# Attention mask built from rows for each bit on GpSimd, without the two bucket products

## What is computed

```
q_bits = (einsum('bhsd,dk->bhsk', q, proj) > 0)        # k_bits likewise
mask   = q_bucket[:, :, :, None] == k_bucket[:, :, None, :]
scores = scale * matmul(q, k.T)
scores = where(mask, scores, -1e9);  scores -= max(scores)
attn   = exp(scores);  attn /= attn.sum() + 1e-9
out    = matmul(attn, v)
```

## Time and profile before

| | |
|---|---|
| runs of the kernel | median 616.67 us (616.35 to 617.31), 3 runs |
| the profiled execution | 616.41 us, span of its instructions 614.7 us |
| granted TensorE clock | 1.000 of full speed |
| busy share of the span | TensorE 98%, its weight loads 82%, VectorE 70%, ScalarE 57%, GpSimd 57% |
| attention stage | from the start to about 240 us |

### The profile page before, as it was taken

The page is one execution under the profiler, slowest core; times in us unless marked ns, Lnnn a source line. Parts: engine busy times, 40 slices in busy tenths (PEclk is TensorE's granted clock), DMA queues, the critical chain, the costliest instruction groups (busy, mean ns, idle before and its releaser), DMA issues.

```text
span 614.7 us, 10917 instructions
## 1 busy us (share of the span) xinstructions
PE 605.4 (98%) x3676; PEld 503.5 (82%) x3676; DVE 431.1 (70%) x689; ACT 347.6 (57%) x700; POOL 349.3 (57%) x337
## 2 busy tenths in 40 slices
PE   7899999999999999999999999999999999999998
PEld 3667777776776776999888999999999999988887
DVE  3988888888888885788676666545677666579920
ACT  3877777777777785354444444335444444264232
POOL 4533434333337756146458988873999999234140
PEclk9999999999999999999999999999999999999999
DMA  6842323233232210001212122113222221100202
GB/s 137 244 118 64 91 66 91 64 90 90 64 90 79 62 46 3 1 2 53 69 51 69 56 64 61 60 57 99 69 85 85 86 86 51 35 1 0 86 19 102
DMA packets 27650, 42.20 MB, mean 69 GB/s; under 512 B 3425, under 2 KB 15713, under 8 KB 27617
## 3 DMA queue, kind: packets, MB, share of 16 engines
q1 hardware_dynamic: 25648, 37.38, 20.9%
q0 software_dynamic: 1728, 4.02, 2.6%
q10 hardware_dynamic: 240, 0.39, 0.3%
HBM read 38.63 MB, written 3.15 MB: 68 GB/s over the span
## 4 chain that ended last, share of the span: by engine, by line
PE 95%; DVE 2%; DMA 1%; ACT 1%; POOL 1%; issue 0%; ACTq 0%; POOLq 0%
PE banks L1882 22%; PE banks L1914 16%; PE banks L1667 12%; PE banks L1684 11%; PE banks L1734 10%; PE banks L1996 5%; PE banks L2012 5%; PE banks L1873 4%; PE banks L1707 2%; PE banks L1818 2%; PE banks L1620 2%; DMA k_raw<-in_k 1%; PE banks L1742 1%; PE banks L1858 1%; PE banks L1626 1%; PE banks L1792 1%
## 5 line engine op out<-in xcount | busy, mean ns | idle before, releaser
L1246 DVE TENSOR_REDUCE row_min<-banks 128x1 f32<-128x768 f32 x96 | 91.8, 956 | 31.8 <-PE banks L1667 31.1
L873 ACT ACTIVATE prob<-banks,row_min 128x768 f32<-128x768 f32 x96 | 87.1, 907 | 29.0 <-DVE row_min L1246 28.9
L1506 DVE TENSOR_TENSOR partial_sums<-banks,partial_sums 128x384 f32<-128x384 f32 x78 | 43.4, 557 | 54.9 <-PE banks L1914 54.7
L1734 PE MATMUL banks<-ident,prob 128*128 128x128 f32 x576 | 79.2, 273 | 1.4 <-ACT probT L374 1.4
L1734 PEld LDWEIGHTS banks<-ident,prob 128*128 128x128 f32 x576 | 68.1, 140 | 6.7 <-issue 1.9
L606 POOL TENSOR_TENSOR k_b<-k_raw,k_a 64x768 fp32r<-64x768 f32 x16 | 29.3, 1829 | 70.7 <-ACT k_a L856 70.7
L1684 PE MATMUL banks<-probT,v_in 128*64 128x384 f32 x384 | 69.0, 494 | 0.0
L1882 PE MATMUL banks<-h_hi,w_hi 128*128 128x512 f32 (+1 forms) x256 | 66.1, 339 | 0.0
L1882 PE MATMUL banks<-h_hi,w_lo 128*128 128x512 f32 (+1 forms) x256 | 65.6, 337 | 0.0
L1882 PE MATMUL banks<-h_lo,w_hi 128*128 128x512 f32 (+1 forms) x256 | 65.3, 336 | 0.0
L374 ACT COPY probT<-banks 128x384 f32<-128x384 f32 x104 | 49.1, 480 | 22.4 <-PE banks L1734 22.1
(11 more groups left out here) (216 smaller groups left out, 1515.0 us busy)
## 6 DMA issues: line engine op xcount, KB each, us to landing
w_stage<-in_moe_w_ch SPq DMA_DIRECT2D x38, 256.0 KB, 2.6
q_raw<-in_q SPq DMA_DIRECT2D x32, 192.0 KB, 3.3
k_raw<-in_k SPq DMA_DIRECT2D x30, 192.0 KB, 3.6
w_pair<-in_moe_w_ch SPq DMA_DIRECT2D x7, 512.0 KB, 3.7
v_in<-in_v SPq DMA_DIRECT2D x16, 192.0 KB, 2.8
w_stage<-in_moe_w_ch SPq DMA_DIRECT2D x6, 512.0 KB, 3.8
out<-y_out SPq DMA_DIRECT2D x11, 256.0 KB, 2.0
seq_tables_sb<-in_dft POOLq DMA_DIRECT2D x6, 386.0 KB, 3.7
```

The costliest lines, as they stand in the source:

```text
L873: act.activation(prob[s % 2][:, :, :], s_tile(s), ACT.Exp, bias=row_min[:, s:s + 1], scale=-1.0, accum_out=row_sum[:, s:s + 1]).then_inc(e ...
L1246: dve.tensor_reduce(row_min[:, s:s + 1], s_tile(s), AX.XY, ALU.min).then_inc(min_ready, 1)
L1506: dve.tensor_tensor(out, product_bank[PRODUCT_BANK[o]], other, ALU.add).then_inc(done, 1)
L1734: op = pe.transpose(bank[:, j * P:(j + 1) * P], prob[tile % 2][:, c, j * P:(j + 1) * P], ident[:, :])
```

## The change

Each of the six bits of q and k now gets two rows in the operands. VectorE writes the bits as 0 and 1 for q and 0 and 2^44 for k (L1234's successor). GpSimd makes from them, for each half of the columns, a row block for q (the bit less an offset) and one for k (an offset less the bit): four instructions of 32 x 384 for each head (`make_mask`). Their products add 2^44 to the score for every bit that differs. The operands have 96 rows in use instead of 128 in the second pair of matmuls. Slots 2, 4, 8 and 10 have no task left.

A row in which no key matches has a minimum of 2^44 or more. A new VectorE instruction in each slot (`shift_and_scale`, 128x2) compares the minimum with 2^43 and gives bias and scale for the exponential: the minimum and -1, or 0 and 0. It waits for the minimum, and ScalarE waits for it.

The projections `w_q`, `w_k` are written twice. Two loads at the start are replaced by smaller ones. The first head's mask is made by VectorE. GpSimd's four mask instructions of a head stand ahead of its subtractions, and in the last pair the folds of rows are put around them; ScalarE's two roundings for the Fourier stage go from slots 6 and 7 to 8 and 9. The last scratch use of a pair takes another bank.

```
-        PREPARE = {0: ["B"], 2: ["C0"], 4: ["C1"], 6: ["B"], 8: ["C0"], 10: ["C1"]}
+        PREPARE = {0: ["B"], 6: ["B"]}
...
+        if banks[-1] == banks[0]:
+            banks[-1] = banks[1]
...
-        prologue = ["B", "C0", "C1"]
+        prologue = ["B"]
...
+        def make_mask(eng, h, chunk):
+
+            cols = slice(chunk * HALF, chunk * HALF + HALF)
+            q_rows = slice(chunk * GROUP, (chunk + 1) * GROUP)
+            k_rows = slice(D + chunk * GROUP, D + (chunk + 1) * GROUP)
+            eng.tensor_tensor(q_b[h][MASK_ROWS, cols], bits_sb[q_rows, :],
+                              bit_offset[q_rows, :].broadcast_to([GROUP, HALF]), ALU.subtract).then_inc(mask_ready, 1)
+            eng.tensor_tensor(k_b[h][MASK_ROWS, cols], bit_offset[k_rows, :].broadcast_to([GROUP, HALF]),
+                              bits_sb[k_rows, :], ALU.subtract).then_inc(mask_ready, 1)
...
-            pool.dma_start(codes[:, :, :], bucket_codes).then_inc(codes_loaded, 16)
+            pool.dma_start(bit_offset[:, :], bucket_ones).then_inc(offset_loaded, 16)
...
+            def masks(i, use):
+
+                h, nxt = head_of_task(i, use)
+                wait_drained(pool, i, use)
+                for chunk in range(2):
+                    make_mask(pool, h, chunk)
+                pool.wait_ge(mask_ready, 4 * (operands(i + nxt, h) + 1))
...
             split_qk(0, 0)
+            pool.wait_ge(offset_loaded, 16)
+            masks(0, (0, "B"))
             split_qk(0, 1)
...
             def prepare_pair(i):
 
+                masks(i - 1, (6, "B"))
                 split_qk(i, 0)
                 scale_q(i, 1)
...
+                masks(i, (0, "B"))
                 split_qk(i, 1)
                 scale_q(i + 1, 0)
...
-            fold_rows(0, slice(0, DM))
+            fold_rows(0, slice(0, DM), (0,))
+            pool.wait_ge(rows_added, HT)
+            masks(NP - 2, (6, "B"))
             split_qk(NP - 1, 0)
             scale_q(NP - 1, 1)
-            pool.wait_ge(fold_edge, 3)
+            fold_rows(0, slice(0, DM), (1,))
+            pool.wait_ge(rows_subtracted, HT)
+            masks(NP - 1, (0, "B"))
+            split_qk(NP - 1, 1)
+            pool.wait_ge(lo_done, 4 * NP)
             fold_first()
             fold_edges(0)
-            split_qk(NP - 1, 1)
...
-                need(act, min_ready, i * SLOTS + (s + 1))
+                need(act, shift_made, i * SLOTS + (s + 1))
...
-                act.activation(prob[s % 2][:, :, :], s_tile(s), ACT.Exp, bias=row_min[:, s:s + 1],
-                               scale=-1.0, accum_out=row_sum[:, s:s + 1]).then_inc(exp_done, 1)
+                act.activation(prob[s % 2][:, :, :], s_tile(s), ACT.Exp, bias=row_shift[:, s, 0:1],
+                               scale=row_shift[:, s, 1:2], accum_out=row_sum[:, s:s + 1]).then_inc(exp_done, 1)
...
-                    if last == 1 and s in (6, 7):
-                        round_parts(0, s - 6)
+                    if last == 1 and s in (8, 9):
+                        round_parts(0, s - 8)
...
+                dve.tensor_scalar(bits_sb[:, :], scratch(i, use), 0.0, bit_size[:, :], ALU.is_gt, ALU.mult)\
+                   .then_inc(scratch_free[bank_of(i, use)], 1)
...
+            def shift_and_scale(i, s):
+
+                dve.wait_ge(min_ready, i * SLOTS + (s + 1))
+                dve.scalar_tensor_tensor(row_shift[:, s, :], row_min[:, s, 0:1].broadcast_to([P, 2]), BIG / 2,
+                                         row_min[:, s, :], ALU.is_lt, ALU.mult).then_inc(shift_made, 1)
...
                         row_minimum(i, s)
+                        shift_and_scale(i, s)
...
+                upper = slice(0, D + GROUP)
+                for lhs, rhs, start in ((q_a[h], k_a[h], True), (q_b[h][upper], k_b[h][upper], False)):
```

More of the change, by code:

```diff
@@ L352, in operands @@
             return i * 2 + h
[L354 to L360, removed]
         def drain_prob(eng, copy, i, use):
@@ L627, in _, with fold_rows @@
             pool.memset(xo[:, :, 0:1], 0.0).then_inc(fold_edge, 1)
-            def fold_rows(b, cols):
-                for n in range(2):
+            def fold_rows(b, cols, which=range(2)):
+                for n in which:
                     for t in range(HT):
@@ L1208, in _ @@
             dve.wait_ge(proj_loaded, 16)
-            dve.wait_ge(consts_ready, 3)
-            dve.tensor_scalar(w_q[top, 0:BITS], proj_sb[:, :], -1.0, None, ALU.mult).then_inc(w_ready, 1)
-            dve.tensor_copy(w_k[top, 0:BITS], proj_sb[:, :]).then_inc(w_ready, 1)
+            dve.wait_ge(consts_ready, 5)
+            twice = proj_sb[:, :].unsqueeze(1).broadcast_to([D, 2, BITS])
+            both = [w[top, 0:2 * BITS].rearrange("p (n c) -> p n c", n=2) for w in (w_q, w_k)]
+            dve.tensor_scalar(both[0], twice, -1.0, None, ALU.mult).then_inc(w_ready, 1)
+            dve.tensor_copy(both[1], twice).then_inc(w_ready, 1)
             dve.wait_ge(top_loaded, 32)
@@ L1307, in pair @@
                         invert_sums(i - 1, 1)
-            for task in prologue:
-                prepare(-1, (0, task))
+            prepare(-1, (0, "B"))
+            dve.wait_ge(offset_loaded, 16)
+            wait_drained(dve, -1, (0, "B"))
+            for chunk in range(2):
+                make_mask(dve, 0, chunk)
             pair(0, 0)
@@ L1622, in bits @@
                 return op
-            def buckets(i, use):
-                return pe.matmul(scratch(i, use), codes[:, int(use[1][1]), :], bits_sb[:, :], start=True, stop=True)
             def wait_free(i, use):
@@ L1634, in prepare @@
                 wait_free(i, use)
-                if use[1] == "B":
-                    if isinstance(i, int) and i < 0:
-                        pe.wait_ge(top_scaled, 1)
-                    else:
-                        need(pe, q_scaled, operands(i + nxt, h) + 1)
-                    op = bits(i, use, h)
-                else:
-                    if use[1] == "C0":
-                        of_head = range(6) if use[0] < 6 else range(6, SLOTS)
-                        wait_drained(pe, i, (0 if isinstance(i, int) and i < 0 else
-                                             next(x for x in of_head if "B" in PREPARE.get(x, [])), "B"))
-                    op = buckets(i, use)
-                op.then_inc(scratch_full[bank_of(i, use)], 1)
+                if isinstance(i, int) and i < 0:
+                    pe.wait_ge(top_scaled, 1)
+                else:
+                    need(pe, q_scaled, operands(i + nxt, h) + 1)
+                bits(i, use, h).then_inc(scratch_full[bank_of(i, use)], 1)
             def scores(i, s):
@@ L1653, in scores @@
                 if qt == 0:
-                    made = [prepared(i, s, task) for task in ("C0", "C1")]
-                    for j, use in {bank_of(j, use): (j, use) for j, use in made}.values():
-                        wait_drained(pe, j, use)
+                    need(pe, mask_ready, 4 * (operands(i, h) + 1))
                     need(pe, hi_done, 3 * operands(i, h) + 3)
@@ L1761, in _ @@
             prepare(-1, (0, "B"))
[L1762 to L1766 removed]
+            for blocks in (3, 3, 3, 3):
                 keep_busy(blocks)
@@ L2086, in bucket_tables @@
     import numpy as np
-    number = np.arange(P - dim)
-    has = (number[None, :] >> np.arange(bits)[:, None]) & 1
-    codes = np.zeros((P, 2, P), np.float32)
-    for chunk in range(2):
-        codes[32 * chunk:32 * chunk + bits, chunk, :dim] = 2 * has - 1
-        codes[64 + 32 * chunk:64 + 32 * chunk + bits, chunk, dim:] = 2 * has - 1
-    ones = np.zeros((P, 1), np.float32)
-    ones[:dim, 0] = ones[dim:, 0] = has.sum(axis=0)
-    return codes, ones
+    size, offset = np.ones((P, 1), np.float32), np.zeros((P, 1), np.float32)
+    size[dim:] = 2.0 ** 44
+    for group in range(0, P, P // 4):
+        if group < dim:
+            offset[group + bits:group + 2 * bits] = 1.0
+        else:
+            offset[group:group + bits] = 2.0 ** 44
+    return size, offset
 _INS = ["q", "k", "v", "proj", "moe_w_ch1", "moe_w_ch2", "moe2_w_val", "moe2_conv_w", "moe2_w_out"]
```

63 lines of the change are left out of this document (24 added, 39 removed).

## The result

The changed kernel takes 640.49 us (median of 4 runs, 637.29 to 641.26), the kernel before beside it 616.79 (616.35 to 617.31). The ratio is 1.037, with a 95% interval of 1.033 to 1.040: slower by 23.7 us. The profiled execution took 637.29 us, with a span of 635.6; against 616.41 before it is 20.9 us longer, and those I account for.

The account below looks back on a forecast made before the run. TensorE sets the pace, with 0.1 us of room in the slot 3 to 5 loop. 14 heads x 0.85 = 11.9, +0.9 first head, +1.2 last head, -0.2 start: +13.8 on 616.4, said 630; range 615.5 to 641.

Parts of the forecast that it names:

- second rival: GpSimd masks shorter than 0.73: k subtraction holds slot 2's instruction to 7.1; 1.6 us a head, 640; chance 0.10, or worse.
- The holds: Attention heads: VectorE's new instruction, two SBUF inputs, waits for running GpSimd instructions; slot 3's to 9.37; head 0.85 us longer.
- first rival: New instruction not held: a head changes by -0.03 to +0.07 us, total 614.5 to 617.5; chance 0.25.
- Bucket products, instruction, scale column, exponential: Prices in a head: two TensorE products of 0.17 removed; VectorE instruction 0.17 plus 0.04 wait, exponential's scale column 0.1 added.
- Masks, 4 x 0.85: Four GpSimd mask instructions a head, 0.85 us each, 2.25 to 5.5 after a head's first scores, then the k subtraction.
- third rival: GpSimd masks at 1.01: q subtraction ends 0.6 later, 1.3 to 1.4 us a head, 636; no chance of its own.
- Slot 1's wait is covered: Slot 1's new instruction, ready 3.4, waits to 3.9 at no cost, since slot 3's scores come after the values.
- It is the masks ahead of it that push it onto the new instruction: GpSimd's q subtraction, before ending with slot 3's minimum, now runs 7.5 to 9.35 and holds the instruction to 9.37.
- The start, -0.2: Kernel start: a 128 KB load replaced by one of 0.5 KB, taken as 0.2 us gained.
- The last head, +1.2: Last attention head: no masks, but GpSimd splits and folds without pause, so 1.2 us longer.

Follow-up runs that it names:

- e1: The changed kernel with the new instruction's minimum and minus one in PSUM, so one SBUF input in place of two: 621.12 us, ratio 1.007.
- e2: The changed kernel without the new VectorE instruction, the exponential's scale constant -1 again, rows without a match unhandled: 613.39 us, ratio 0.995.
- e11: The changed kernel with row_den and its reciprocal moved from slots 2 and 8 to slots 6 and 0: 643.72 us, ratio 1.044.
- e12: The changed kernel with GpSimd's order k subtraction, q subtraction, masks, scaling, where the masks came first: 631.82 us, ratio 1.025.
- e3: The changed kernel with GpSimd's masks cut from 384 to 8 columns after the first head: 631.27 us, ratio 1.024.
- e4: The kernel before with only the new VectorE instruction and the scale column added, no masks on GpSimd: 633.80 us, ratio 1.027.
- e10: The changed kernel with the minimum and the first head's bits in PSUM and a sixth of the values in slot 4: 617.95 us, ratio 1.0021.
- e9: The changed kernel with a sixth of a head's values moved to slot 4, parts of 3, 1 and 2 key tiles: 635.45 us, ratio 1.030.
- e6: The changed kernel with TensorE's values in three equal parts at slots 0, 2 and 4: 642.04 us, ratio 1.042.
- e8: The changed kernel with the minimum in PSUM, values over slots 0, 2, 4, first head's masks by tensor_scalar with one SBUF data input: 620.95 us.

## Why the prediction was right, and where it was off

It forecast a slower kernel by way of held VectorE instructions, 630.2 us for an execution that took 637.3. The direction and the mechanism came out; the size was too small by a third or more (+13.8 where the profiled execution has +20.9 and the medians +23.7). That 640.49 still lies half a microsecond inside the range owes to luck: the range reached up that far for the second rival (masks so short that the k subtraction holds slot 2's instruction), which the changed kernel doesn't show. By its own steps:

- **The holds.** Right. e1 shows it: the same work with one SBUF input in place of two, no hold of the new instruction, -19.4 us. The first rival (not held, 614.5 to 617.5) is out. Even e1's head is 0.20 longer than before, where that rival's sum gave -0.03 to +0.07: it counted only the loop from slot 3 to slot 5 (3.22, in e1 3.38) and not that TensorE's values ahead of it and transposes behind it then also take longer (2.16 for 2.09, 0.77 for 0.66).
- **Bucket products, instruction, scale column, exponential.** 0.30 of 0.34 gained (e2), 0.16 for my 0.17, 0.09 for my 0.1.
- **Masks, 4 x 0.85: the step that was mis-sized in the steady head.** One takes 0.82, but they start 0.90 apart, and the k subtraction begins 0.17 after the last. From the end of a head's first scores (135.08) it starts at 6.00, not 5.5. All that I listed behind it came in its order and as late: k subtraction to 7.83 (7.35), row_den to 7.86 (7.35), q subtraction to 9.74 (9.35), minimum 8.00 to 8.96 (7.55 to 8.50), instruction to 9.75 (9.37), exponential from 9.87 (9.48), end of the scores of slot 5 at 11.96 (11.61). These are the numbers of the head shown above; the head of the earlier trace rows itself has 5.99, 9.74 and 11.90 in their place. So the scores of slot 5 end 1.18 later than before for my 0.89, and a head took 1.13 more for my 0.85. Over 14 heads: 15.85 for 11.9. My third rival, which had the masks at 1.01 each and said 1.3 to 1.4 a head and 636, is slightly nearer in size for that reason.
- **"Slot 1's wait is covered".** The scores of slot 3 did come 0.5 us late, because the values wait for a transposed copy behind the held instruction (5.0 us in all in the waits). But it cost nothing, since slot 3's instruction was held to the q subtraction's end anyway; e11 shows it, where that instruction starts 0.7 us earlier against this end and gains nothing.
- **"It is the masks ahead of it that push it onto the new instruction".** The larger part of it. With the masks last (e12) 0.75 of the 1.15 us goes. Of the 0.40 that stays, half is still there when nothing holds the instruction (e1), and half is a hold by the q subtraction, which later exponentials delay (e3, e4).
- **The start, -0.2.** This step failed: it was +0.5 in this execution. GpSimd's first subtraction did begin sooner, at 8.11 for 9.23, and the masks took that back and more. In the other kernels whose first masks are made in the same way the first scores start at 13.54 to 14.30, so 0.5 is near the low end. I held the new instruction to GpSimd's lock and forgot the first head's four masks, which I had VectorE make with two SBUF inputs: 1.04 and 2.05 us for the first two, 0.55 for the two behind the last subtraction. e10, with the bits in PSUM, has the first minimum back at its old place.
- **The last head, +1.2.** It was +4.0: one hold of 2.41 us across two GpSimd instructions, TensorE idle for 2.27 of them, and then 3.4 us at the lower clock. I had holds there at 1.2 in all and the clock at nothing.

Sum: 15.85 (11.9) + 0.6 (0.9) + 4.0 (1.2) + 0.5 (-0.2) = 20.9, where I had 13.8. Five other executions of the changed kernel are on record: 636.9 us at a mean granted clock of 1.000, and 639.9 to 641.3 at 0.989 to 0.994, where this one had 637.3 at 0.997. That the extra 3 us are more low-clock stretches is likely by that; no trace of those executions shows it. The profiled executions of e1, e2 and e9 show one such stretch that this one lacks, in the first head after TensorE had been idle for over 3 us.

## What to carry to other kernels

Before a small VectorE instruction goes between two engines that wait for each other, look at where its data inputs lie and at what GpSimd runs just then: here 0.16 us became 0.37 in the median and 2.41 at the worst, and with the minimum in PSUM it was 0.22 always. When two engines hold each other, GpSimd's busy share (63%) says nothing about slack: its chain of masks and subtractions, by the hold at its end, became the path of the head, and then cover on TensorE gave 5 us at best (e9; e6 lost 1.6) and freeing another held instruction (e11) nothing, while taking work off that chain (e12) gave 8.7 and cutting the link (e1) 19.4. And price a chain of small instructions by start to start, not by their durations.

## What the runs showed of the hardware

- The hold isn't only a matter of two SBUF inputs. A tensor_scalar with one SBUF input of data and a column took 1.92 us beside a GpSimd subtraction, 0.41 without (e8). row_den, a tensor_scalar with one SBUF input and no column, took 1.61 beside one and 0.17 without. With the input in PSUM it was 0.61 to 0.63 beside the same subtractions (e10). The Trainium skill (SBUF — State Buffer, "Who interferes with whom") says so of VectorE's two-port modes, for which tensor_scalar is eligible, and these rows agree.
- A held instruction need not get its turn when one GpSimd instruction ends: at 245.03 it waited through the end of one split at 246.20 and all of the next, to 247.42, which began without a gap. Between masks, with 0.07 us from end to start, it got it at once (139.15). The traces of all the kernels here say the same of the new instruction and row_den. In 360 places a GpSimd instruction ended while one of the two was held and the next began at least 0.07 us later; the held one was through within 0.04 us each time. In 94 places the next began without a gap, and in 45 of them it waited on. What decides between these isn't shown.
- That held instruction cost its own stretch, and then TensorE's clock: after 2.27 us of standing still the granted clock was 0.79 in the 5 us that hold the stop and 0.87 in the next 5, and matmuls took 1.01 for 0.62.
- On TensorE a scores group behind a values group took 0.90 us and behind transposes 0.70 to 0.79, so cutting one group of values in two cost 0.26 us.
